# The softmax gate moved from the expert layer's hidden rows to the output rows of the feed-forward

## The reference, cut to what matters

```python
# mixture layer: x [1792, 768], 8 experts, w1 [8, 768, 1024], w2 [8, 1024, 768]
logits = (x / (norm(x) + 1e-6)) @ (emb / (norm(emb) + 1e-6)).T / tau
expert = argmax(logits);  probs = softmax(logits, with 1e-9 added to the sum)
gate   = probs[row, expert[row]]
y[row] = gate * (relu(x[row] @ w1[expert]) @ w2[expert])
# feed-forward: w_in [768, 2048], w_out [2048, 768]
h = y @ w_in
out = max(0.01 * h, h) @ w_out
```

## Time and profile before

| what | value |
|---|---|
| median of 3 runs | 1298.55 us (1298.49 to 1299.23) |
| profiled execution | 1300.97 us, its span 1299.2 us |
| PE busy | 1213.4 us (93%), 6978 matmuls |
| DVE, ACT, POOL busy | 887.5, 738.4, 699.3 us |
| mean granted TensorE clock | 0.981 |

### The profile page before, as it was taken

How to read it: one execution, slowest core, us unless ns; L and a number is a source line. 1 busy time by engine, 2 the same in 40 slices (tenths; PEclk the granted TensorE clock), 3 DMA queues, 4 the chain that set the end, 5 groups by cost and what they waited for, 6 DMA issues and landing times. The chain is left out here.

```text
span 1299.2 us, 21341 instructions
## 1 busy us (share of the span) xinstructions
PE 1213.4 (93%) x6978; PEld 1061.5 (82%) x6978; DVE 887.5 (68%) x1167; ACT 738.4 (57%) x1419; POOL 699.3 (54%) x797
## 2 busy tenths in 40 slices
PE   4999999999589999999999987999999999999996
PEld 3888888888478888878888776999999999999995
DVE  5999999998759999999999993545322245551222
ACT  5999999999457877878778772222221122221110
POOL 7998888884659999999999981000001001000012
PEclk9999999999689999999999998999999999999999
DMA  2244434221135435444454022121322212212221
GB/s 68 73 132 109 112 97 108 73 65 41 36 122 202 154 131 188 147 178 148 159 205 140 32 94 90 49 61 50 98 73 78 87 55 86 61 37 55 57 90 55
DMA packets 99501, 126.62 MB, mean 97 GB/s; under 512 B 30328, under 2 KB 79224, under 8 KB 99392
## 3 DMA queue, kind: packets, MB, share of 16 engines
q1 hardware_dynamic: 94240, 103.14, 26.0%
q0 software_dynamic: 5152, 22.12, 4.7%
HBM read 187.68 MB, written 19.34 MB: 159 GB/s over the span
## 5 line engine op out<-in xcount | busy, mean ns | idle before, releaser
L959 ACT CAST w_hi<-w_raw 128x768 fp32r<-128x768 f32 (+1 forms) x294 | 251.8, 934 | 5.5 <-DMA x_rows<-logits 4.6
L1458 POOL DMA_INDIRECT out_rows<-o_sb,out_index x23 | 22.4, 973 | 317.4 <-DVE o_sb L1579 317.1
L1158 DVE TENSOR_TENSOR w_lo<-w_raw,w_hi 128x1024 fp32r<-128x1024 f32 x82 | 175.1, 2163 | 7.3 <-ACT w_hi L959 7.3
L1166 DVE TENSOR_TENSOR w_lo<-w_raw,w_hi 128x768 fp32r<-128x768 f32 x126 | 159.9, 1327 | 4.1 <-ACT w_hi L959 4.1
L1551 DVE TENSOR_TENSOR w_lo<-out_raw,w_hi 128x384 fp32r<-128x384 f32 x64 | 35.7, 558 | 170.9 <-ACT w_hi L1489 170.9
L1394 PE MATMUL ps_acc<-gT_hi,w_hi 128*128 128x448 f32 x384 | 143.0, 372 | 0.0
L1395 PE MATMUL ps_acc<-gT_hi,w_lo 128*128 128x448 f32 x384 | 141.1, 367 | 0.0
L1396 PE MATMUL ps_acc<-gT_lo,w_hi 128*128 128x448 f32 x384 | 141.1, 367 | 0.0
L1489 ACT CAST w_hi<-out_raw 128x384 fp32r<-128x384 f32 x64 | 32.8, 513 | 187.4 <-PE ps_acc L1396 187.1
L1483 ACT ACTIVATE small_h<-ps_acc 128x448 f32<-128x448 f32 x64 | 34.9, 546 | 181.4 <-PE ps_acc L1366 181.4
L876 PE MATMUL ps_h<-w_hi,xT_hi 128*128 128x512 f32 x252 | 103.0, 409 | 25.5 <-POOL w_lo L764 14.8
(11 more groups left out here) (224 smaller groups left out, 3238.7 us busy)
## 6 DMA issues: line engine op xcount, KB each, us to landing
w_raw<-moe_w_in SPq DMA_DIRECT2D x80, 1536.0 KB
in_raw<-moe_w_in_in SPq DMA_DIRECT2D x32, 384.0 KB, 3.4
out_raw<-moe_w_out_in SPq DMA_DIRECT2D x64, 192.0 KB, 2.3
qk_raw<-q_in SPq DMA_DIRECT2D x48, 112.0 KB, 2.0
qk_raw<-k_in SPq DMA_DIRECT2D x48, 112.0 KB, 2.1
v_raw<-v_in SPq DMA_DIRECT2D x48, 112.0 KB, 2.0
x_rows<-x_tok SPq DMA_DIRECT2D x48, 112.0 KB, 2.6
w_raw<-moe_w_in SPq DMA_DIRECT2D x6, 512.0 KB, 4.3
```

What stands on the lines that cost most here:

```text
L959: act.copy(out[:, c, :], raw[:, c, :]).then_inc(s_hi, 1)
L1158: dve.tensor_tensor(w1_lo[:, c, :], w1_raw[:, c, :], w1_hi[:, c, :].bitcast(F32), ALU.subtract).then_inc(s_w1lo, 1)
L1166: dve.tensor_tensor(w2_lo[:, c, :], w2_raw[:, c, :], w2_hi[:, c, :].bitcast(F32), ALU.subtract).then_inc(s_w2lo, 1)
```

## The change

1. The gate is no longer made in `experts`: `square_x`, `exponent`, `top`, `exp` and `gate_of` are gone there, and `relu` has no scale and no wait for the gate.
2. The row numbers of column 768 are written by ACT (`row_id`, behind the high parts of w2) from a float copy `slot_id`, not by POOL.
3. `h_lo` of the last item goes ahead of four low parts of w2 on DVE; the first tile of y may be transposed before the last item's ReLU and split are done; four tiles are transposed two chunks earlier.
4. The last item's indirect store is issued by POOL as its first act in `feed_forward`, behind the block's end. The loads of y wait for it there.
5. `feed_forward` loads column 768 of all rows of y in one transfer (`ids`, 14 values in each of 128 partitions), makes the row numbers of the output from it, gathers the rows of x again by those numbers (14 tiles of 128 rows, three buffers inside `oT`), sums their squares on ACT between the hidden steps of the first half, keeps the logits on POOL, and makes 14 columns of gates with a few instructions spread over the first output pass.
6. DVE's copy of an output tile out of PSUM becomes a multiplication by the tile's column of gates (line 1579).
7. `load_in(2)` is issued first on SP, ahead of the wait for the stores of y.

```diff
@@ experts, POOL: store_y @@
             def store_y(n, u):
                 pool.wait_ge(s_yc, n + 1)
-                pool.tensor_copy(y_sb[u][:, DM:DM + 1], slot_in[:, n:n + 1]).then_inc(s_id, 1)
                 pool.wait_ge(s_id, n + 1)
@@ experts, POOL @@
             def body(n, u):
                 if n >= 2:
-                    lo2(n - 1, pool2(n - 1)[:1])
-                gate_of(n)
-                if n >= 2:
-                    lo2(n - 1, pool2(n - 1)[1:])
+                    lo2(n - 1, pool2(n - 1))
                     store_y(n - 2, u)
                 if n + 2 < items:
                     gather(n + 2, u)
                 if n + 1 < items:
                     lo1(n + 1)
-                    exponent(n + 1)
...
             lo2(items - 1, pool2(items - 1))
-            for j in range(TILES):
-                index(j)
             store_y(items - 2, items % 2)
-            store_y(items - 1, (items - 1) % 2)
@@ experts, ACT @@
             def relu(n, half):
-                act.wait_ge(s_gate, n + 1)
-                act.activation(h_sb[:, half * H1:(half + 1) * H1], ps_h[:, half, 0:H1], ACT.Relu, scale=gate[:, n:n + 1]).then_inc(s_relu, 1)
+                act.activation(h_sb[:, half * H1:(half + 1) * H1], ps_h[:, half, 0:H1], ACT.Relu).then_inc(s_relu, 1)
...
+            def row_id(n, u):
+                if n > 1:
+                    act.wait_ge(s_y_out[u], uses(n - 2, u))
+                act.copy(y_sb[u][:, DM:DM + 1], slot_id[:, n:n + 1]).then_inc(s_id, 1)
...
                 if n >= 2:
-                    for c in range(C2 // 2):
+                    for c in range(C2):
                         hi2(n - 1, c)
-                exp(n, u)
-                if n >= 2:
-                    for c in range(C2 // 2, C2):
-                        hi2(n - 1, c)
+                    row_id(n - 2, u)
                 relu(n, 0)
@@ experts, DVE @@
                 if more:
                     x_lo(n + 1)
-                    top(n + 1, 1 - u)
                     for c in range(C1 // 2):
                         lo1(n + 1, c)
-                else:
+                h_lo(n, u)
+                if not more:
                     for c in range(C2 // 2):
                         lo2(n, c)
-                h_lo(n, u)
@@ experts, PE: between the chunks of the last product2 @@
-                if 3 <= c < TILES:
-                    transpose_tile(c)
+                if 3 <= c + 2 < TILES:
+                    transpose_tile(c + 2)
@@ feed_forward, SP @@
+            load_in(2, 2, 0)
+            for u in range(2):
+                sp.wait_ge(s_y_out[u], stored[u])
+            sp.dma_start(ids[:, :], y_rows[0:N, DM:DM + 1].rearrange("(j p) o -> p (j o)", p=P), allow_slow_non_contiguous=True).then_inc(s_ids, 16)
@@ feed_forward, POOL @@
+            def gather_x(t):
+                if t >= K:
+                    pool.wait_ge(s_xss, t - K + 1)
+                    pool.wait_ge(s_lg, t - K + 1)
+                pool.indirect_dma_start(out=x_tile[t % K], out_offset=None, in_=x_rows,
+                                        in_offset=bass.IndirectOffsetOnAxis(ap=out_index[:, 2, t:t + 1], axis=0)).then_inc(s_xg[t % K], 16)
+            def keep_logits(t):
+                pool.wait_ge(s_xg[t % K], 16 * (t // K + 1))
+                pool.tensor_copy(logits[:, t, :], x_tile[t % K][:, DM:X]).then_inc(s_lg, 1)
...
+            last = items - 1
+            pool.indirect_dma_start(out=y_rows, out_offset=bass.IndirectOffsetOnAxis(ap=slot_rows[:, last:last + 1], axis=0),
+                                    in_=y_g[last % 2][:, :], in_offset=None).then_inc(s_y_out[last % 2], 16)
+            index()
+            for t in range(K):
+                gather_x(t)
+            for t in range(J):
+                keep_logits(t)
+                if t + K < J:
+                    gather_x(t + K)
+            exponents()
+            guard_sums()
...
+            def square_x(t):  
+                act.wait_ge(s_xg[t % K], 16 * (t // K + 1))
+                act.activation(x_tile[t % K][:, 0:DM], x_tile[t % K][:, 0:DM], ACT.Square, accum_out=x_ss[:, t:t + 1]).then_inc(s_xss, 1)
...
                 for f in range(G - 2):
                     scale_h(f + at, f % 2)
                     in_high(f + (at + 2), f % 2)
+                    if hf == 0 and f > 0:
+                        square_x(f - 1)
@@ feed_forward, DVE: copy_out @@
-                dve.tensor_copy(out_buffers[out_slot(tile)], ps_tr[:, tile % 2, 0:K * P]).then_inc(s_o, 1)
+                if tile == 0:
+                    dve.wait_ge(s_gate, 1)
+                row = TILES * (tile // TILES // 2) + tile % TILES
+                dve.tensor_scalar(out_buffers[out_slot(tile)], ps_tr[:, tile % 2, 0:K * P], denom[:, row:row + 1], None, ALU.mult).then_inc(s_o, 1)
```

More of the change, by code:

```diff
@@ L645, in experts @@
         in_item_ranked = sb("in_item_ranked", [R, J, cols], F32R)
-        x_ss, x_norm, x_more, x_inv, neg_top, shift, denom, denom_more, gate = (
-            sb(x, [P, items]) for x in ("x_ss", "x_norm", "x_more", "x_inv", "neg_top", "shift", "denom", "denom_more", "gate"))
-        exps = [sb(f"exps{u}", [P, E]) for u in range(2)]
-        ones_f, eps_f, tiny_f = sb("ones_f", [P, 1]), sb("eps_f", [P, 1]), sb("tiny_f", [P, 1])
         ps_x = ctx.enter_context(nc.psum_tensor("ps_xm", [P, 2, 512], F32))
@@ L1041, in _ @@
                 hi2(items - 1, c)
+            row_id(items - 2, items % 2)
             for j in range(TILES):
@@ L1044, in _ @@
             in_high()
+            row_id(items - 1, (items - 1) % 2)
         @block.vector
@@ L1267, in sem @@
             return ctx.enter_context(nc.semaphore(name))
-        y_g, out_index = shared["y_sb"], shared["out_index"]
+        y_g, slot_rows = shared["y_sb"], shared["slot_rows"]
+        items = slot_rows.shape[1]
+        ids, out_index = sb("ids", [P, J]), sb("out_index", [P, 3, J], I32)
+        x_ss, top, denom, logits = sb("x_ss", [P, J]), sb("top", [P, J]), sb("denom", [P, J]), sb("logits_f", [P, J, E])
         yT_hi, yT_lo = shared["w1_hi"][:, :, 0:W], shared["w1_lo"][:, :, 0:W]
@@ L1457, in store @@
                 row, dh = TILES * (n_pass // 2) + j, n_pass % 2
-                pool.indirect_dma_start(out=out_halves, out_offset=bass.IndirectOffsetOnAxis(ap=out_index[:, row, dh:dh + 1], axis=0),
+                pool.indirect_dma_start(out=out_halves, out_offset=bass.IndirectOffsetOnAxis(ap=out_index[:, dh, row:row + 1], axis=0),
                                         in_=out_buffers[out_slot(tile)], in_offset=None).then_inc(s_store[out_slot(tile)], 16)
-            for j in range(TILES):
-                index(j)
-            pool.wait_ge(s_idx, TILES)
+            last = items - 1
[10 more added lines that the diff above has]
+            guard_sums()
             for tile in range(4 * TILES):
@@ L1598, in _ @@
                         out_low(f + base, f % 2)
+                        if n_pass == 0 and f == 2:
+                            tops()
+                        if n_pass == 0 and f == 6:
+                            sum_exps()
+                        if n_pass == 0 and f == 9:
+                            gates()
                         if 3 <= f < TILES + 3:
```

133 lines of the change are left out of this document (62 added, 71 removed).

## The result

The kernel after takes 1248.97 us (median; 1247.97 to 1249.28), the one before 1298.89 beside it (1298.49 to 1300.18). The ratio is 0.9613, with a 95% interval from 0.9596 to 0.9629: 49.9 us less, where 37.5 were forecast, and 0.03 us under the range. The profiled execution has 1249.2 us and a span of 1247.4.

A forecast was written before the change was run, and what follows sets the result against it. PE, DVE and POOL were close to full in the experts' items, PE stalling 2.1 us per item through the gate's chain and low parts. Savings 25.8 + 3.0 + 7.2 + 1.5 = 37.5 from 1298.55 gave 1261 us, range 1249 to 1283.

The forecast's parts named there:

- The item: Experts' steady part, 17 items: without the gate the cycle falls from 20.32 to DVE's 18.8 us, saving 25.8 us.
- The standing: Experts' items: DVE's low parts stand still behind POOL's for 5.8 of DVE's 18.8 us per item, taken as unchanged.
- PE's floor: Rival for the experts' items: PSUM readers lie beside POOL, PE's own cycle binds; 47.6 us saved, 1251 us, chance 0.16.
- the first door: Experts' items: PE's 2.1 us stall per item comes partly through the gate's chain, ACT waiting 57.2 and 21.6 us for POOL.
- The low parts and DVE: Experts' items: DVE's low parts of weights and POOL's exclude each other; POOL's take 8.3 us per item, DVE's own work 13.0.
- `row_id` on ACT: Experts' items: ACT replaces POOL's cast at no cost while ACT has slack; without it at most 15 us.
- End of the experts: Last item: `h_lo` ahead of four low parts removes PE's wait before the tile transposes; gain 3.0 us, between 0 and 4.9.
- block's end: Between experts and feed-forward: PE's 8.7 us wait, fitted by the last scatter, falls to 1.5; gain 7.2 us.
- clock: Feed-forward's first matmuls: the higher clock level throughout instead of half clock after the idle time; gain 1.5 us, lower bound 0.
- The DRAIN: POOL's drain at the block's end, 5.06 us before, fits a wait for the last scatter; forecast under 1 us after.
- next late: End of the experts: after `h_lo`, the tile's own load and `copy_y(19)`, behind three more low parts of DVE, are late.
- The feed-forward: Gate's work moved there (`ids`, gathers, squares, gates) costs nothing, bounded by 6 us if `ids` takes twice its upper estimate.

The follow-up runs named there:

- the last run: Kernel after with another DVE order in the last item alone (last but one copy of y and first four tiles' low parts earlier): 1246.02 us, ratio 0.9593.
- e_pool2_three: Kernel after with three of the eight low parts of w2 on POOL where there were two: 1270.49 us, ratio 0.9772.
- e_dummy_add: Kernel after with six small POOL instructions per item put back on private columns, each an addition instead of a power: 1282.17 us, ratio 0.9858.
- e_act_free: Kernel before with ACT freed of both waits for POOL, ReLU unscaled and exponential reading constants: 1292.38 us, ratio 0.9937.
- e_relu_free: Kernel before with the ReLU's wait for the gate and its scale taken out, gate still computed: 1299.83 us, ratio 1.0.
- e_cast_back: Kernel after with the row id of items 0 to 19 written by POOL again, ahead of its scatter: 1258.77 us, ratio 0.9685.

## Why the prediction came out as it did

**The item (25.8 forecast, 37.4 measured) is the step that failed.** It said: "Were DVE's idle time all gone and the standing unchanged, the cycle would be DVE's 18.8". The idle time went as said: 1.30 us by the rows in order of time, 0 after (but not with the gate's chain: with that alone cut it was still 1.17). The standing, the time that DVE's low parts stood behind POOL's, did not stay: DVE's busy time fell from 19.0 to 18.1 us. POOL's low parts beside anything but DVE's own low parts rose from 0.72 + 0.99 = 1.71 to 2.60, 0.9 us more, which is that fall. (I had put the first of these at 2.5, as the rest of a sum.) I had priced the removal of POOL's small instructions only through the waits that they caused, and at nothing as work, because POOL did not look like the bound. The runs showed the reverse: the waits of ACT alone 8.7 us (some 12 at an even clock), the six instructions alone 27.9 (25.5 in the items), the seventh one (the cast) 9.8. These don't add up to 37.4, since PE's 18.1 us is a floor under all of them. The rival "PE's floor" was right, in mechanism too: low parts beside the PSUM readers, 2.6 of 3.1 us.

**The waits.** That the gate's chain was the first door was a misreading of the earlier trace rows: 57.2 and 21.6 us were the longest waits, but of an engine that had time to spare. Taking the smaller one away gave nothing in the whole time, and both together 8.7 us.

**The low parts and DVE.** That they exclude each other, save where DVE reads PSUM, was right: DVE's 50 PSUM readers in the kernel after kept their length. That the run with three parts came within 0.1 us of an item was in part luck, since its mean is made of items of 18.1 to 26.7 us. The rule of the Trainium skill ("SBUF — State Buffer", section "Who interferes with whom") agrees with the 1.21 us of `h_lo` beside POOL's low part at 553.70. Read by that rule alone, the prediction would have given 1251 and not 1261, the better number here, since I had bounded the overlap by the state of the kernel before, the one thing that the change moved.

**`row_id` on ACT** costs nothing that shows, and is worth 9.8 us against POOL, which I had not counted.

**End of the experts (3.0) and block's end (7.2): 10.2 against 10.9; clock: 1.5 against 1.6.** The wait at the block's end fell from 8.73 to 1.32 on the two traces, 7.4; 5.6 of it is the scatter, by the run with the scatter put back, and the rest a `copy_y` that began 1.6 us behind PE's last product before and right behind it now. The clock's gain lies in the feed-forward: the tenth matmul there started 3.48 us behind the first before, 1.90 after. The scatter with its clock measured 7.1 by the medians (7.2 + 1.5 forecast for all of it). The other 3.5 us, forecast as 3.0, came, but not from the order of the last item, which is worth nothing. That product1(20) and what follows gained from running without POOL's small work, like the items, is likely and not shown: the stretch is 37.8 us with the six powers put back, but 35.0 with six additions. The DRAIN, forecast under 1 us, took 6.8 and cost nothing, since it began early. What I named as next late, `copy_y(19)` behind three more low parts, was so, 1.41 us, and the last run took it away.

**The feed-forward (0, at most 6).** No PE wait in the hidden stage, and the first rows of x were there 15 us into it (13 to 21 forecast). The gate's work costs 1.2 us in POOL's DRAIN at the kernel's end, which the prediction did not name; the scaled copies cost nothing that shows. It was shorter all the same: by 3.0 us, which are 1.1 in the first hidden stage (the clock's 1.6 is in it) and 3.4 in the output's passes, which the prediction had at nothing, less 1.5 at the end. The likely reason for the passes' 3.4 is where their tiles lie.

Additions cost what powers do, but for the clock that fell in their items; why it fell there and hardly with powers stays open. No run moved a PSUM reader alone, so that the overlap is the cause rests on the table's sums; what is shown is that POOL's small instructions are the main cost, since six of them alone bring 25.5 of the items' 37.4 us back. Which address makes the output's matmuls faster was not tried.

## What to carry to other kernels

A long wait names a late engine, not a price: take it away alone before you count on it, and give the suspected work back alone to see what it costs. Where two engines shut each other out except in some instructions and no third one is slower, the cycle is their sum less what falls beside those instructions, and one-column work in front of a heavy instruction can move that by a microsecond. The scatter that the block's end waited for cost 5.6 us of waiting and some 1.5 of the clock behind it: issue such a one behind the barrier, with work in front of its reader.

## What the hardware showed unexpectedly

One unused tile of 812 bytes per partition, with nothing else changed, made the last 576 matmuls of the output's passes follow each other every 0.205 us and not every 0.210 (117.7 and 120.6 us from the first to the last), and those of the second hidden stage every 0.208 and not every 0.207 (119.8 and 118.8).

A low part of DVE that stands behind POOL does not come in between POOL's: one stood for 11.63 us behind five of them in e_pool2_three, where it takes 1.21 alone.

In the middle of the items, with PE at work on both sides, the granted clock fell to 0.50 for 3.4 us at a time in four kernels, at waits of PE such as 2.08 us (e_dummy_add), 2.28 (e_act_free), 2.42 (e_relu_free) and 2.69 (e_cast_back). In three of them such an item took 1.1 to 1.9 us more than the one like it without a fall. So before two such kernels are compared, the granted clock of the stretch has to be.

A POOL instruction on one column takes 0.65 us (addition) or 1.01 (power) at the mean among DVE's low parts. In the kernel before with its powers made additions, `x_more`, which stands right behind another small one, took 0.19 every time (count, duration ns min/median/max):

```profile
L780 POOL TENSOR_TENSOR x_more<-x_norm,eps_f x15: 189/190/190, 433.9 to 703.9; 128x1 f32<-128x1 f32 x15
```

A drain of POOL took 6.8 us here and 9.8 with another order of the last item, both without cost, since DVE's ended later. At the kernel's end, where nothing hides it, it took 2.35 us before and 3.57 after.
